# Attention output of a gated linear attention kernel computed transposed, with the diagonal term moved into the masked scores

## What is computed

```
for t in range(S):
    cur = u * k[t] (outer) v[t]
    y[t] = r[t] @ (state + cur)
    state = w[t][:, None] * state + k[t] (outer) v[t]
```

## Time and profile before

| | before |
|---|---|
| median of 3 runs | 1093.19 us (1089.14 to 1094.92) |
| profiled execution, its own time | 1092.39 us |
| its span | 1090.5 us |
| PE busy / weight loads | 96% / 92% of the span |
| DVE / ACT / POOL busy | 68% / 48% / 20% |
| granted TensorE clock, mean | 0.985 of full |

### The profile page before, as it was taken

One profiled execution on the slowest core, in us unless ns is written; L12 is line 12 of the kernel. 1 busy time (PEld: TensorE's weight loads), 2 busy tenths in 40 slices (PEclk: granted clock), 3 DMA queues, 4 the chain that ended last, 5 costly groups with the idle time before them and its releaser, 6 DMA issues.

```text
span 1090.5 us, 19839 instructions
## 1 busy us (share of the span) xinstructions
PE 1049.7 (96%) x7543; PEld 1001.0 (92%) x7543; DVE 738.4 (68%) x1406; ACT 519.4 (48%) x901; POOL 219.8 (20%) x205
## 2 busy tenths in 40 slices
PE   5999899999999999999999899999999999999995
PEld 4776699999999999999999899999999999999995
DVE  4687676887887887864566667577585657667570
ACT  2343233343333343333355366567575656556571
POOL 0000000101101101101221523423433432422331
PEclk9899999999999999999999999999999999999998
DMA  9786533368344455011276788888797878889751
GB/s 230 176 176 161 136 55 61 54 69 96 68 56 62 91 53 70 13 35 50 80 173 118 184 242 249 249 222 259 221 299 207 256 228 244 251 228 295 212 158 15
DMA packets 197890, 166.36 MB, mean 153 GB/s; under 512 B 129874, under 2 KB 181460, under 8 KB 197796
## 3 DMA queue, kind: packets, MB, share of 16 engines
q1 hardware_dynamic: 184820, 144.78, 53.0%
q0 software_dynamic: 12976, 20.32, 9.4%
HBM read 141.21 MB, written 25.22 MB: 153 GB/s over the span
## 4 chain that ended last, share of the span: by engine, by line
PE 81%; DMA 2%; DVE 2%; issue 1%; POOL 1%; ACT 1%; POOLq 0%; ACTq 0%; DVEq 0%
PE bank L789 18%; PE pp L1211 18%; PE bank L1195 17%; PE fx L805 9%; PE yu L221 3%; PE yu L1254 3%; PE pp L183 2%; PE tr L168 2%; PE tr L1176 2%; PE yu L202 1%; PE yu L218 1%; PE yu L1236 1%; DMA slot_entry<-entry,slot_i 1%; PE fx L1236 1%; PE tr L192 1%
## 5 line engine op out<-in xcount | busy, mean ns | idle before, releaser
L789 PE MATMUL bank<-xh,w12h 128*128 128x256 f32 x576 | 167.8, 291 | 1.3 <-DVE ab_all L869 1.3
L789 PE MATMUL bank<-xl,w12h 128*128 128x256 f32 x576 | 163.6, 284 | 0.0
L789 PE MATMUL bank<-xh,w12l 128*128 128x256 f32 x576 | 163.4, 284 | 0.0
L1109 POOL DMA_INDIRECT result<-x2s,who x55 | 93.1, 1693 | 277.1 <-ACT x2s L1328 242.5
L1315 DVE SCALAR_TENSOR_TENSOR abl<-bank,abh 128x512 fp32r<-128x512 f32 x96 | 66.2, 690 | 109.9 <-ACT abh L1310 109.9
L966 POOL DMA_INDIRECT slot_entry<-entry,slot_i x48 | 49.2, 1026 | 399.4 <-DVE token_f L957 388.2
L789 PEld LDWEIGHTS bank<-xh,w12h 128*128 128x128 f32 x576 | 111.2, 193 | 2.5 <-DVE ab_all L869 2.5
L789 PEld LDWEIGHTS bank<-xl,w12h 128*128 128x128 f32 x576 | 111.3, 193 | 0.0
L789 PEld LDWEIGHTS bank<-xh,w12l 128*128 128x128 f32 x576 | 110.9, 193 | 0.0
L1195 PE MATMUL bank<-xh,set_up_h 128*128 128x256 f32 x384 | 109.2, 284 | 0.2 <-DVE abl L1315 0.2
L1195 PE MATMUL bank<-xh,set_up_l 128*128 128x256 f32 x384 | 108.6, 283 | 0.0
(11 more groups left out here) (235 smaller groups left out, 2804.3 us busy)
## 6 DMA issues: line engine op xcount, KB each, us to landing
up_raw<-in_moe_w SPq DMA_DIRECT2D x93, 512.0 KB, 4.6
down_raw<-in_moe_w SPq DMA_DIRECT2D x124, 384.0 KB, 5.0
padded<-in_w SPq DMA_DIRECT2D x32, 144.0 KB, 4.3
padded<-in_k SPq DMA_DIRECT2D x32, 144.0 KB, 4.9
padded<-in_r SPq DMA_DIRECT2D x32, 144.0 KB, 4.2
vs<-in_v SPq DMA_DIRECT2D x32, 144.0 KB, 3.4
attention_out<-ys SPq DMA_DIRECT2D x32, 144.0 KB, 2.0
result<-zeros SPq DMA_DIRECT2D x3, 1536.0 KB
```

Of the source, the lines that this page charges most:

```text
L789: last = nc.tensor.matmul(bank[f % 2][:, m * TG:(m + 1) * TG], wp[:, m, kk, f * P:(f + 1) * P], xp[:, kk, :], start=(n == 0), stop=(n == 3 ...
L1109: nc.gpsimd.indirect_dma_start(out, bass.IndirectOffsetOnAxis(who[v % 4][:, s, 0:1], 0), yo[v % 2][:, s, 0:DM], None, bounds_check=N - 1, ...
```

## The change

1. `pe_output` swaps its operands. The state is stationary and `rdec` moves (128 columns, not 96); the values are stationary, padded to 64 columns a head, and `att` moves (128 columns, not 48). Head h writes PSUM partitions 64h to 64h+63. `yu` has features on the partitions and time in the columns.
2. The diagonal goes into `att` before the mask: ScalarE writes `ident` scaled by `diag` into `att` (`act_spread`, 12 instructions of 128x128 a pair), and `dve_mask` becomes a predicated copy of the scores over it, where `causal` is set. `dve_diag_values` and `dve_output` are gone; ScalarE copies `yu` out (`act_output`).
3. `attention_out` is features x tokens. A half is stored with two DMAs of 48 rows; the dense stage loads a group with features on the partitions. `pe_turn` is gone; `act_turn` and `dve_turn` read the loaded tile in SBUF.
4. `added` has two buffers, padding columns of `vs` and `state` are set to zero by POOL at the start, `u` is loaded earlier, and the steps for the diagonal move one pair ahead.

```diff
 def sp_attention_store(sp, b, q, half):
-            sp.dma_start(xa[bass.ds(b * S + half * S // 2, S // 2), 2 * D * q:2 * D * (q + 1)].rearrange("(c p) j -> p c j", p=C),
-                         ys[i][:, 3 * half:3 * half + 3, :]).then_inc(y_stored[i][half], 16)
+            for h in range(2):
+                sp.dma_start(xa[D * (2 * q + h):D * (2 * q + h + 1), bass.ds(b * S + half * S // 2, S // 2)],
+                             yt[half][h * HB:h * HB + D, :]).then_inc(y_stored[half], 16)
 def pe_output(pe, b, q, half):
                 if c:
-                    nc.tensor.matmul(yu[:, o:o + 96], rdec[q % 2][:, c * C:(c + 1) * C], state[:, c - 1, :],
-                                     start=True, stop=False, skip_group_check=True)
+                    nc.tensor.matmul(yu[:, t], state[:, c - 1, :, :].rearrange("p h x -> p (h x)"),
+                                     rdec[q % 2][:, c * C:(c + 1) * C], start=True, stop=False, skip_group_check=True)
                 for h in range(2):
-                    last = nc.tensor.matmul(yu[:, o + h * D:o + (h + 1) * D], att[:, c // 2, h, c % 2, :],
-                                            vs[q % 2][:, c, h, :], start=(c == 0), stop=True,
-                                            skip_group_check=True)
+                    last = nc.tensor.matmul(yu[h * HB:(h + 1) * HB, t], vs[q % 2][:, c, h, :], att[:, c // 2, h, c % 2, :],
+                                            start=(c == 0), stop=True, skip_group_check=True)
+        def act_spread(act, b, q, j):
+            g = HP * b + q
+            if j == 0:
+                act.wait_ge(diag_ready, g + 1)
+                need(act, yu_full, 3 * g)
+            for h in range(2):
+                for c in range(2):
+                    last = nc.scalar.activation(att[:, j, h, c, :], ident[:, :], ACT.Copy, scale=diag[:, 2 * j + c, h:h + 1])
+            last.then_inc(spread_ready, 1)
 def dve_mask(dve, b, q, j):
-            nc.vector.tensor_tensor(att[:, j, :, :, :],
-                                    pp[:, :, 0:2 * C].rearrange("p h (c x) -> p h c x", c=2),
...
-                                    ALU.mult).then_inc(att_ready, 1)
+            nc.vector.copy_predicated(att[:, j, :, :, :],
...
+                                      pp[:, :, 0:2 * C].rearrange("p h (c x) -> p h c x", c=2)).then_inc(att_ready, 1)
-        def dve_diag_values(dve, b, q):
...
-        def dve_output(dve, b, q, half):
...
+        def act_output(act, b, q, half):
+            g = HP * b + q
+            need(act, y_stored[half], 32 * g)
+            act.wait_ge(yu_full, 3 * g + 2 + half)
+            nc.scalar.copy(yt[half][:, :], yu[:, 0:S // 2]).then_inc(y_ready, 1)
 def pair_slots(q):
-            return [[("score", q, 0), ("keys", q, 0), ("diag", q, 2)],
-                    [("score", q, 1), ("in", q + 1, 0), ("diag", q, 3)],
-                    [("score", q, 2), ("state", q, 0)],
+            return [[("score", q, 0), ("keys", q, 0), ("diag", q + 1, 0)],
+                    [("score", q, 1), ("in", q + 1, 0), ("diag", q + 1, 1)],
+                    [("score", q, 2), ("state", q, 0), ("diag", q + 1, 2)],
...
-                    [("derive", q + 1, 3)], [("derive", q + 1, 4), ("derive", q + 1, 5)],
-                    [("diag", q + 1, 0)], [("diag", q + 1, 1)]]
+                    [("derive", q + 1, 3), ("spread", q + 1, 0)],
+                    [("derive", q + 1, 4), ("derive", q + 1, 5), ("spread", q + 1, 1)],
+                    [("spread", q + 1, 2)], []]
-        def pe_turn(pe, b, q, part):
...
 def act_turn(act, b, q, part):
-            nc.scalar.copy(xh[:, slice(*TURN[part]), :], turned(part)).then_inc(xh_ready, 1)
+            nc.scalar.copy(xh[:, two, :], tokens_of(q)[:, two, :]).then_inc(xh_ready, 1)
 def sp_group_load(sp, b, q):
-                sp.dma_start(xr[q][:, :, :], xa[bass.ds(b * S + q * TG, TG), :].rearrange("(s p) d -> p s d", p=P)
+                sp.dma_start(tokens_of(q), xa[:, bass.ds(b * S + q * TG, TG)].rearrange("(k p) t -> p k t", p=P)
```

More of the change, by code:

```diff
@@ L95, in program @@
         padded = [asb(f"padded{i}", [P, 3, NC, 2, HB]) for i in range(2)]
-        vs = [asb(f"vs{i}", [P, NC, 2, D]) for i in range(2)]
+        vs = [asb(f"vs{i}", [P, NC, 2, HB]) for i in range(2)]
         wt, kt, rt = asb("wt", [P, S]), asb("kt", [P, S]), asb("rt", [P, S])
@@ L103, in program @@
         att = asb("att", [P, 3, 2, 2, C])
-        added = asb("added", [P, NC - 1, 2 * D])
-        state = asb("state", [P, NC - 1, 2 * D])
+        added = [asb(f"added{i}", [P, NC - 1, 2 * D]) for i in range(2)]
+        state = asb("state", [P, NC - 1, 2, HB])
         diag = asb("diag", [P, NC, 2])
-        diag_v = asb("diag_v", [P, NC, 2, D])
-        ys = [asb(f"ys{i}", [P, NC, 2 * D]) for i in range(2)]
+        yt = [asb(f"yt{half}", [P, S // 2]) for half in range(2)]
         attn_end = nc.sbuf_base
         xr_loaded = [asem("xr_loaded0")]
-        consts_ready, ident_ready, padded_clear, small_loaded = (sem(x) for x in ("consts_ready", "ident_ready", "padded_clear", "small_loaded"))
+        consts_ready, ident_ready, padded_clear, small_loaded, pad_zero = (sem(x) for x in ("consts_ready", "ident_ready", "padded_clear", "small_loaded", "pad_zero"))
         ones_ready, cleared = sem("ones_ready"), sem("cleared")
@@ L415, in act_attention @@
                 act_state(act, b, q)
+            elif step == "out":
+                act_output(act, b, q, n)
+            elif step == "spread":
+                act_spread(act, b, q, n)
             elif step == "keys":
@@ L434, in dve_attention @@
                 dve_products(dve, b, q, n)
-            elif step == "diag" and n == 2:
+            elif step == "diag":
                 dve_diag(dve, b, q)
-            elif step == "diag":
-                dve_diag_values(dve, b, q)
             elif step == "state":
                 dve_state(dve, b, q)
-            elif step == "out":
-                dve_output(dve, b, q, n)
         def sp_attention(sp, b, step, q, n):
@@ L455, in program, with tokens_of @@
         TURN = ((0, 2), (2, KD))
-        def turned(part):
-            lo, hi = TURN[part]
-            return bank[part][:, 0:(hi - lo) * TG].rearrange("p (k t) -> p k t", k=hi - lo)
-        def pe_turn(pe, b, q, part):
-            i = NG * b + q
-            if part == 0:
-                pe.wait_ge(xr_loaded[q], 16 * (b + 1))
-            need(pe, ab_free, KF * i - 1 + part)
-            if part == 1 and q == 0 and b:
-                need(pe, place_free, i - 1)
-            for kk in range(*TURN[part]):
-                for s in range(ST):
-                    last = nc.tensor.transpose(turned(part)[:, kk % 2, s * P:(s + 1) * P],
-                                               xr[q][:, s, kk * P:(kk + 1) * P], ident[:, :])
-            last.then_inc(turn_full, 1)
+        def tokens_of(q):
+            return xr[q][:, :, :].rearrange("p s d -> p (s d)").rearrange("p (k t) -> p k t", k=KD)
         def act_turn(act, b, q, part):
             need(act, ab_full, KF * (NG * b + q))
-            act.wait_ge(turn_full, 2 * (NG * b + q) + part + 1)
-            nc.scalar.copy(xh[:, slice(*TURN[part]), :], turned(part)).then_inc(xh_ready, 1)
+            if part == 0:
+                act.wait_ge(xr_loaded[q], 16 * (b + 1))
+            two = slice(*TURN[part])
+            nc.scalar.copy(xh[:, two, :], tokens_of(q)[:, two, :]).then_inc(xh_ready, 1)
         def dve_turn(dve, b, q, part):
@@ L614, in _ @@
                                             base=0, pattern=[[1, P]], channel_multiplier=-1).then_inc(consts_ready, 1)
+                    for i in range(2):
+                        nc.gpsimd.memset(vs[i][:, :, :, D:HB].rearrange("p c h x -> p (c h) x"), 0.0).then_inc(pad_zero, 1)
+                    nc.gpsimd.memset(state[:, :, :, D:HB].rearrange("p c h x -> p (c h) x"), 0.0).then_inc(pad_zero, 1)
                     nc.gpsimd.memset(zeros[:, :], 0.0).then_inc(zeros_ready, 1)
@@ L699, in _ @@
                     pe.wait_ge(wal_ready, KF)
-                    for part in range(2):
-                        pe_turn(pe, 0, 0, part)
         with ExitStack() as ph:
@@ L1186, in pe_hidden @@
                         pe.wait_ge(ab_free, KF * GROUPS)
-                if v < 2 and m == 1 - v:
+                if v < 2 and m == 0:
                     pe.wait_ge(place_free, GROUPS - 1 + v)
@@ L1588, in group @@
                         bb, q = of_group(b, q)
-                        if step == "turn":
-                            pe_turn(pe, bb, q, n)
-                        elif step == "up":
+                        if step == "up":
                             pe_up(pe, bb, q, n)
```

91 lines of the change are left out of this document (35 added, 56 removed).

## The result

The changed kernel takes 1095.08 us in the median of 20 runs (1091.95 to 1100.04), the kernel before 1091.49 (1087.56 to 1094.92, also 20). The ratio is 1.0031, with an interval from 1.002 to 1.0042: by it 3.4 us slower (the medians differ by 3.6), which is less than half a per cent and is counted here as no change. The profiled execution of the changed kernel took 1096.20 us, 3.8 more than the one of before.

The account below looks back on a forecast made before the run. TensorE's queue was taken to bound the kernel; +8 - 8 - 0.7 + 0.9 + 1 = +1.2 us on the profiled 1092.4, which lies 0.8 under the median, gave 1094.5 us, with an eight-in-ten range of 1083 to 1113.

Parts of the forecast that it names:

- The output on TensorE: Output matmuls: 96 switches between whole array and column halves cost more than overlapping heads save; +8 us, +1 to +13.
- 0.755 us: One output chunk on TensorE after the change, switches and unhidden loads included, against 0.67 before; charged for 96 chunks.
- half of 0.107: Second pair of values matmuls in a chunk: saving from loading 64 stationary columns, not 128, if loads go by columns.
- up to 0.075: Output chunk, after the switch back to whole array: extra us for the first load, which isn't hidden; an estimate.
- The transposes: Turn transposes on TensorE, six in each of 12 groups at 0.65 to 0.70 us, disappear; -8 us.
- The change of stage: Casts before the next stage: xh starts without the turn; saves 1.3 us, 0.65 already in the transposes; -0.7 us.
- The start: Kernel start: u issued before wo takes 0.93 us of the queue, and TensorE waits for gates behind wo; +0.9 us.
- ScalarE and VectorE: Mixed stage: ScalarE's added work mostly hidden, +1 us, up to +10; VectorE's lost work and predicated copy have room.
- the first: Rival, output matmuls: no switch cost between whole array and column halves; -22 us, 1064 to 1065; chance 0.12.
- the second: Rival, values matmuls: heads don't overlap in column halves, or switches are dearer; +21 us, 1115; chance 0.12.
- the third: Rival, dense steps: ScalarE's bundles delay copy a_sb; 0.3 us x 48 bundles, 14 us, 1105 to 1110; chance 0.10.
- The fourth: Rival, mixed stage: VectorE's relief removes TensorE's waits and late multiplications in dense steps; -6 us, 1088; chance 0.06.

Follow-up runs that it names:

- e5: Changed kernel with each half's state matmuls before its values matmuls, accumulation flags set to keep all states; 1079.10 us, 0.9851 to the kernel before.
- e8: The changed kernel run again, unedited, on the second chip of the follow-ups; 1099.56 us, 1.0048 to the kernel before.
- e12: The changed kernel run a third time, unedited, on the third chip of the follow-ups; 1103.09 us, 1.0051 to the kernel before.
- part 2 alone: Kernel before with only ScalarE's diagonal activations, predicated copy, ScalarE's output copy and earlier diagonal steps; TensorE's work unchanged; run twice, 1.0069 and 1.0051 to before.
- e6: Changed kernel with three of four diagonal activations per bundle removed for every pair but the first; 1097.91 us, 1.0023 to the kernel before.
- e9: e5 with the diagonal written into att by VectorE, 48 multiplications in place of 192 ScalarE activations; 1080.97 us, 0.9852 to the kernel before.
- e2: Changed kernel with values matmuls on the whole array, one head's values beside zeros, added in one buffer; 1095.79 us, 0.9974 to the kernel before.
- e7: The kernel before, unchanged, profiled for one execution on one of the follow-up chips; 1096.98 us.
- e1: Changed kernel with each half's state matmuls before its values matmuls, part of the states left out of the output; 1087.15 us, 0.9888 to the kernel before.
- e3: Changed kernel with the load of u back behind the values of the first pair; 1104.06 us, 1.0039 to the kernel before.
- e4: First run of part 2 alone on the kernel before, on the first chip of the follow-ups; 1103.62 us, 1.0069 to the kernel before.
- e10: Second run of part 2 alone on the kernel before, on the third chip of the follow-ups; 1104.63 us, 1.0051 to the kernel before.

## Why the prediction was right

**The output on TensorE** (forecast +8 us, from +1 to +13). From start to start it was 59.3 us before and 67.2 after: +7.9. That the total is so close is luck, since two errors cancel. A chunk behind another one was forecast at 0.755 us and took 0.79, so +0.12 and not +0.085. But the forecast charged all 96 chunks alike, and the 16 chunks without a state became 0.11 shorter, while the first chunk of a second half grew by 0.08 only (0.60 to 0.68). The mechanism held in each piece: in 0.20 and out 0.20 as the scores' rows said, pairs in step. The load of 64 columns is shorter; by line and engine in e5:

```profile
L222 PEld LDWEIGHTS yu<-att,vs x384: 132/137/138, 43.1 to 481.6; 128*64 128x64 f32 x192
```

137 ns where 128 columns take 192 (L217 and the page's PEld groups): 55 less. The forecast had taken off half of 0.107, 53. The length of a load's record doesn't go by columns alone, though: the 128-column loads of the transposes (L472) take 141. In the starts of e5 the second pair of values comes 0.153 after the first, the scores' second pair 0.22. What was too small is the term for the load behind the switch back: "up to 0.075", of which the sum of 0.755 held all; measured, the second state instruction comes 0.213 to 0.22 after the first, 0.11 late. The Trainium skill, "TensorEngine Tiling (Array Packing)", section Tiling Modes, says that only a change of mode, not of tile, drains TensorE. The trace agrees for columns as well as rows: within the twelve values instructions of e5 the heads alternate at no cost, 0.81 us for all, and each change to or from the whole array costs.

**The transposes** (-8): 72 instructions fewer. From start to start they held TensorE 5.6 us in the 11 groups behind the first, 0.51 a group; the forecast had added durations, whose ends are modelled. Behind such a block the next matmul came up to 0.10 later than usual, twice a group, which would bring a group to the 0.65 to 0.70 of the forecast. So the term lies between -6 and -8.

**The change of stage** (-0.7 beside them). The timeline of the changed kernel, to be held against the earlier trace rows:

```profile
127.64 0.49 ACT L583 CAST wah<-bank 128x400 fp32r<-128x400 f32 x1 [3.27 <-PE bank L679]
128.03 0.93 ACT L462 CAST xh<-xr 128x512 fp32r<-128x512 f32 x2
128.17 0.57 DVE L615 TENSOR_TENSOR wal<-bank,wah 128x400 fp32r<-128x400 f32 x1 [4.37 <-ACT wah L583]
128.69 1.03 DVE L468 TENSOR_TENSOR xl<-xr,xh 128x512 fp32r<-128x512 f32 x2
...
130.18 0.86 PE L182 MATMUL pp<-rdec,kdiv 48*128 48x128 f32 x8 [2.58 <-PEq L500]
```

From `wah` to the next stage 2.54 us, before 3.96: 1.4 less, forecast 1.3.

**The start** (+0.9). It was +1.8: the wait on the gates ends at 14.90, before at 13.11. The queue was not what made it so: `wo` was issued 0.8 later (at 5.30, before at 4.51), but the gate matrix that TensorE waits for at the same time (6.61, before 6.58), and its transfer took 8.2 us to land for 6.5. The forecast had half of the size and the wrong place.

**ScalarE and VectorE** (+1 and nothing). The bundle of four took 1.28 us (forecast 1.3), the predicated copy 0.73 (between 0.69 and twice that; the lower end):

```profile
L308 ACT ACTIVATE att<-ident,diag 128x128 f32<-128x128 f32 x192 | 61.0, 394 | 0.0
...
L316 DVE COPY_PREDICATED att<-causal,pp 128x512 f32<-128x512 int32 x48 | 35.2, 734 | 33.1 <-PE pp L182 32.9
```

In the profile of the changed kernel TensorE's waits on them grew by 1.1 us in sum (`x2s` 1.5 to 2.2, the states 3.3 to 3.6, the masks 2.0 to 2.1). That is the size that was forecast, but not the place: the waits on `ab_all`, behind the bundles, stayed at 1.3 us.

**The sum.** With the terms as measured, +7.9 for the output, -5.6 for 11 groups of transposes, -1.4 for the change of stage with the first group in it, +1.8 for the start and +1.1 for these waits, it is +3.8, and the profiled executions differ by 3.8, the medians by 3.6. That it closes is luck too. The transposes' term may be 2 us larger, and a term is missing: the clock. The mean granted clock was 0.987 and 0.985 before, and the kernel before had a stretch at the lower clock between 80 and 100 us (mean 0.91) that the changed kernel didn't have (1.00), worth 1.8 us. So 2 us or more of the time are in none of these terms, and where they lie wasn't found. In e8 and e12, too, less was lost to the clock than in the kernel before on their chips (0.9870 against 0.9859, 0.9862 against 0.9847), by 1.1 and 1.5 us.

What the sum doesn't explain is part 2 alone at 5.6 to 7.6 us. In the changed kernel the same part sits inside 3.4 to 5.6 in all, so its price is not a fixed one that adds to the others. Stops without a named releaser and the lower clock that followed account for some of it in the two profiles; whether the part brings them is open. A profile of before and of part 2 from many executions on one chip would tell; it wasn't made.

Of the rivals, the first (no switch for columns, 1064) and the second (no overlap, 1115) are refuted by the timeline; the third in its stated form, 14 us, by e6 and e9 and by the waits on `ab_all`, which stayed at 1.3 us; a few us of it stay possible. The fourth didn't show, as the waits of the earlier trace rows stayed.

## What to carry to other kernels

A matmul that uses half of the array has two prices beside its own: the switch in and out, and the first load on each side, which nothing hid here. That came to 0.34 us an excursion (the chunk's 0.79 less 0.45: two state instructions of 0.112 and two pairs of 0.107 to 0.112, with no switch at all), more than the 0.22 that the overlap of two heads saves in four instructions. Chunk 0, which stayed in one form, became cheaper. Put all matmuls of one shape behind each other before judging a layout: the same instructions in another order made 1.0048 into 0.9851. And take the price of an unmeasured form from the nearest measured one in the trace, part by part; the scores' rows gave each piece of it within 0.04 us. Then multiply each kind of chunk by its own number: the first of a row and one in the middle don't cost the same.

## What was not expected of the hardware

Engines stood still for 2 to 7.7 us with no releaser that the profile names, on ScalarE above all (in e2 three waits before `a_sb` come to 14.5 us), at places that differ from kernel to kernel but in part come back. ScalarE stood at 302 to 310 us in seven profiles (the changed kernel's three, e1, e2, e3, e5), and at 422 to 441 in eight, the kernel before in e7 (432 us) among them. In e1 and e5, whose order is the same, the longest wait of TensorE for a mask was 3.4 us, at 225 us, behind such a stop of ScalarE; in e4 and e10, which are one kernel, it was 2.4 to 2.5 us, at 234. Their cause was not found.
